# Attention levels in 64x64 quarters of the TensorE array, read from the queries themselves, and MLP operations placed ahead of the attention's in each slot

## The reference

```python
# attention: q, k, v, f_logit are (4 batches, 8 heads, 768 tokens, 48 dims)
f = sigmoid(f_logit)
for t in range(768):
    state = f[t][:, None] * state + outer(k[t], v[t])      # 48 x 48 per head
    y[t] = q[t] @ state
x = y as (3072 tokens, 384)
h = x @ w_in                                               # 384 -> 2048
g = where(h >= 1, h, where(h <= -1, 0, (h + 1)**2 / 4));  x = g @ w_out
out = (silu(x @ w_gate) * (x @ w_val)) @ w2_out            # 384 -> 1536 -> 384
```

## Time and profile before

| | |
|---|---|
| median of 3 runs | 1079.31 us (1077.73 to 1080.30) |
| the profiled execution | 1078.47 us |
| its span, first to last instruction | 1076.7 us |
| outside the span | 1.8 us |
| prologue, until the first MLP starts | 0 to 77.6 us |
| first MLP with the attention of units 1 to 5 | 77.6 to 626 us |
| second MLP | 626 to 1076.7 us |
| busy: PE, DVE, ACT, POOL | 1015.5, 547.0, 445.2, 450.8 us |

### The profile page before, as it was taken

How to read it: one execution, slowest core, us unless ns; L and a number is a source line. 1 busy time by engine, 2 the same in 40 slices (tenths; PEclk the granted TensorE clock), 3 DMA queues, 4 the chain that set the end, 5 groups by cost and what they waited for, 6 DMA issues and landing times.

```text
span 1076.7 us, 19206 instructions
## 1 busy us (share of the span) xinstructions
PE 1015.5 (94%) x7816; PEld 828.8 (77%) x7816; DVE 547.0 (51%) x745; ACT 445.2 (41%) x808; POOL 450.8 (42%) x368
## 2 busy tenths in 40 slices
PE   2477899999999999999999999999999999999997
PEld 2465677778778777877788888888888888888886
DVE  7965965884686488568736532223222222222221
ACT  3439538544753855375336532122222222222221
POOL 3956962763564476447327422121221212212121
PEclk9569999999999999999999999999999999999999
DMA  9423005003300600220043110010010010000000
GB/s 357 158 72 145 1 2 216 31 2 124 122 1 2 216 30 2 82 107 2 2 177 131 45 39 22 1 59 1 1 59 1 1 59 1 30 1 1 30 1 29
DMA packets 17367, 63.52 MB, mean 59 GB/s; under 512 B 1920, under 2 KB 2176, under 8 KB 16512
## 3 DMA queue, kind: packets, MB, share of 16 engines
q1 hardware_dynamic: 17280, 62.30, 15.8%
HBM read 52.85 MB, written 9.44 MB: 58 GB/s over the span
## 4 chain that ended last, share of the span: by engine, by line
PE 83%; issue 5%; DVE 5%; ACT 3%; POOL 3%; DMA 1%; SPq 0%; POOLq 0%; ACTq 0%; DVEq 0%
PE acc L445 10%; PE acc L447 10%; PE acc L446 10%; PE bank L473 7%; PE bank L471 7%; PE bank L472 7%; PE hid L431 6%; PE bank L344 5%; PE hid L432 5%; PE hid L433 5%; DVE scores L748 3%; PE hid L473 2%; PE hid L472 2%; PE hid L471 2%; PE bank L376 2%
## 5 line engine op out<-in xcount | busy, mean ns | idle before, releaser
L939 POOL TENSOR_TENSOR g_lo<-prod,g_hi 128x512 fp32r<-128x512 f32 x72 | 93.1, 1293 | 347.4 <-ACT g_hi L650 347.4
L932 POOL TENSOR_TENSOR g_lo<-act_tmp,g_hi 128x512 fp32r<-128x512 f32 x96 | 140.5, 1463 | 188.8 <-ACT g_hi L611 188.8
L837 DVE TENSOR_TENSOR sig<-sig,bank 128x512 f32<-128x512 f32 x72 | 49.6, 688 | 275.9 <-ACT sig L644 275.9
L748 DVE COPY_PREDICATED scores<-mask,bank 64x512 f32<-64x512 int32 x144 | 134.2, 932 | 28.4 <-PE bank L344 26.6
L650 ACT CAST g_hi<-prod 128x512 fp32r<-128x512 f32 x72 | 44.9, 624 | 247.6 <-PE acc L447 247.6
L892 POOL TENSOR_TENSOR keys<-keys,gates 128x512 f32<-128x512 f32 x82 | 110.2, 1343 | 44.1 <-PE bank L344 32.7
L611 ACT CAST g_hi<-act_tmp 128x512 fp32r<-128x512 f32 x96 | 59.6, 621 | 164.1 <-DVE act_tmp L825 164.1
L344 PEld LDWEIGHTS bank<-right_q,keys 128*64 128x64 f32 x2304 | 81.0, 150 | 58.8 <-issue 54.6
L344 PE MATMUL bank<-right_q,keys 128*64 128x64 f32 x2304 | 91.0, 238 | 36.0 <-ACT right_q L546 28.1
L445 PE MATMUL acc<-g_hi,wout_hi 128*128 128x512 f32 x288 | 117.0, 406 | 8.0 <-POOL g_lo L932 8.0
L431 PE MATMUL hid<-x_hi,win_hi 128*128 128x512 f32 x288 | 119.0, 413 | 4.0 <-DVE act_tmp L825 4.0
(11 more groups left out here) (80 smaller groups left out, 1851.6 us busy)
## 6 DMA issues: line engine op xcount, KB each, us to landing
gates<-in_f_dram SPq DMA_DIRECT2D x12, 512.0 KB, 5.3
queries<-in_q_dram SPq DMA_DIRECT2D x12, 512.0 KB, 5.4
keys<-in_k_dram SPq DMA_DIRECT2D x12, 512.0 KB, 4.7
values<-in_v_tok_dram SPq DMA_DIRECT2D x6, 1024.0 KB, 8.8
q_tok<-in_q_tok_dram SPq DMA_DIRECT2D x12, 384.0 KB, 8.6
k_tok<-in_k_tok_dram SPq DMA_DIRECT2D x12, 384.0 KB, 9.0
x_dram<-x_out SPq DMA_DIRECT2D x6, 768.0 KB, 3.9
x_raw<-x_dram SPq DMA_DIRECT2D x6, 768.0 KB, 5.5
```

Source lines behind the costliest of these rows:

```text
L748: last = dve.copy_predicated(o, level_mask(li, half), t[rows(half), :].rearrange("p (x b r) -> p x b r", x=BP, r=m))
L932: pool.tensor_tensor(g_lo[:, c % RING, :], act_tmp[:, 2 + c % 2, :], g_hi[:, c % RING, :].bitcast(F32), ALU.subtract).then_inc(g_lo_done, 1)
```

## The change

The two groups of a level become one visit: `level(a, li)` issues all 16 pairs. Each matmul now contracts over the 64 partitions of one head e, takes its weights (`keys`) and its moving columns (`queries`, every second block of m tokens, or the right half at m = 64) straight from those tensors, and writes 32 columns (64 at m = 64) of 64 partitions; head e goes to its own PSUM bank. That makes 64 matmuls a level (32 at m = 64), each in one of four 64x64 quarters of the array, in turn. `right_q`, its copies on ACT, its clearing and the semaphore `q_copied` go. `scale_q` now waits for the level's matmuls, since they read `queries`; `take_level` takes one head of all pairs rather than one group of both heads. The two last levels, whose blocks need no mask, are taken by ACT (four copies a level, 32 or 64 partitions x 512) and no longer by DVE. The levels have slots 1, 4, 7, 10, 13, 16, 18 (unit 1: 6, 9, 12, 14, 16, 18, 20), and what follows them comes one slot earlier. In each chunk `split_g1`, `activate` and `clamp` now stand before slot 2c, and `square(c)` behind slot 2c of its own chunk.

```diff
-DVE_A_UNIT, ACT_A_UNIT = STEPS + 2, B
+MASKED = 2 * (NL - 2)
+DVE_A_UNIT, ACT_A_UNIT = MASKED + 2, STEPS - MASKED + B
...
 USUAL = Plan(own=(-9, -8), diag=(-8, -7), place=(-6, -5, -4, -3), sigmoid=(-2, -1), gated=(-1, 0),
-             step=(1, 3, 5, 7, 8, 9, 10, 12, 13, 14, 15, 17, 18, 19), last_merge=21,
-             y=(21, 21, 22, 22), y_out=(21, 22, 22, 23), tk=(23, 23, 24, 24), tk_out=(24, 24, 25, 25),
-             kv=25, state=26, state_place=27)
+             level=(1, 4, 7, 10, 13, 16, 18), y=(20, 20, 21, 21), y_out=(20, 21, 21, 22),
+             tk=(22, 22, 23, 23), tk_out=(23, 23, 24, 24), kv=24, decay=21, state=25, state_place=26)
...
-        def level(a, s):
-            li, g = s // 2, s % 2
-            free(a, s)
-            pe.wait_ge(q_copied, a * STEPS + s + 1)
+        def level(a, li):
+            m = LEVELS[li]
+            for e in range(2):
+                free(a, 2 * li + e)
+            pe.wait_ge(q_scaled, a * SCALED_A_UNIT + 2 + 2 * li)
             if li:
-                pe.wait_ge(k_scaled, a * STEPS + s - 1)
+                pe.wait_ge(k_scaled, a * STEPS + 2 * li)
...
+            for x in range(BP):
+                for half in range(2 if li < NL - 1 else 1):
+                    for e in range(2):
+                        t = slice(half * HALF, (half + 1) * HALF)
+                        if li < NL - 1:
+                            o = of(a, 2 * li + e)[rows(half), x * HALF // 2:(x + 1) * HALF // 2]
+                            q_right = queries[rows(e), x, t].rearrange("p (b s r) -> p b s r", s=2, r=m)[:, :, 1, :]
...
+                        last = pe.matmul(o, keys[rows(e), x, t], q_right, start=True, stop=True)
+            last.then_inc(filled, 2)
...
-        def copy_right(a, s):
...
+        def take_level(a, li, e):      # ACT, levels m = 32 and 64
+            act.wait_ge(filled, fill(a, 2 * li + 2))
+            act.wait_ge(dve_took, a * DVE_A_UNIT + MASKED)
...
         def scale_q(a, s):
-            dve.wait_ge(q_copied, a * STEPS + s + 1)
+            dve.wait_ge(filled, fill(a, 2 * li + 2))
...
         def attention(a, h):           # DVE
-            for s in steps_at(a, h - 1):
-                take_level(a, s)
-            for s in steps_at(a, h):
-                scale_q(a, s)
+            for li in levels_at(a, h - 1):
+                if li < NL - 2:
+                    take_level(a, li, 1)
+            for li in levels_at(a, h):
+                for g in range(2):
+                    scale_q(a, 2 * li + g)
+                if li < NL - 2:
+                    take_level(a, li, 0)
...
         for m in range(UNITS):         # DVE; ACT and POOL alike
             for c in range(FC1):
-                for a, place in turns(m, 2 * c):
-                    attention(a, place)
                 if m > 0 or c > 0:
                     activate(*((m, c - 1) if c else (m - 1, FC1 - 1)))
                 clamp(m, c)
+                for a, place in turns(m, 2 * c):
+                    attention(a, place)
                 for a, place in turns(m, 2 * c + 1):
                     attention(a, place)
```

More of the change, by code:

```diff
@@ L65, with levels_at @@
 Q = P // 4
-def steps_at(a, h):
-    return [s for s in range(STEPS) if PLANS[a].step[s] == h]
+def levels_at(a, h):
+    return [li for li in range(NL) if PLANS[a].level[li] == h]
 def turns(m, h):
@@ L350, in level @@
-            last.then_inc(filled, 1)
+                for g in range(2):
+                    pe.wait_ge(k_in[g], 16 * (a + 1))
+            for x in range(BP):
[5 more added lines that the diff above has]
+                            q_right = queries[rows(e), x, t].rearrange("p (b s r) -> p b s r", s=2, r=m)[:, :, 1, :]
+                        else:
+                            o = of(a, 2 * li + e)[rows(x % 2), x // 2 * HALF:(x // 2 + 1) * HALF]
+                            q_right = queries[rows(e), x, HALF:P]
+                        last = pe.matmul(o, keys[rows(e), x, t], q_right, start=True, stop=True)
@@ L404, in attention @@
         def attention(a, h):
[L405 to L406 removed]
+            for li in levels_at(a, h):
+                level(a, li)
             for b in range(B):
@@ L526, in place_diag @@
             last.then_inc(diag_placed, 1)
-        def copy_right(a, s):
[L529 to L537, removed]
-                if li < NL - 1:
[L539 to L543, removed]
-                else:
-                    i = i[:, :, HALF:P].rearrange("p x (s t) -> p x s t", s=2)
-                last = act.copy(o, i)
-            last.then_inc(q_copied, 1)
+        def take_level(a, li, e):
+            act.wait_ge(filled, fill(a, 2 * li + 2))
+            act.wait_ge(dve_took, a * DVE_A_UNIT + MASKED)
+            t = bank[fill(a, 2 * li + e) % 3]
+            for half in range(2):
+                if li < NL - 1:
+                    r = slice(half * HALF, half * HALF + HALF // 2)
+                    o = scores[r, :, e, (2 * half + 1) * HALF // 2:(half + 1) * HALF]
+                    last = act.copy(o, t[r, :].rearrange("p (x i) -> p x i", x=BP))
+                else:
+                    o = scores[rows(0), half::2, e, HALF:P]
+                    last = act.copy(o, t[rows(half), :].rearrange("p (x i) -> p x i", x=BP // 2))
+            last.then_inc(act_took, 1)
         def take_keys(a, b):
@@ L575, in attention @@
                     sigmoid(a, g)
-            for s in steps_at(a, h + 1):
-                copy_right(a, s)
+            for li in levels_at(a, h):
+                if li >= NL - 2:
+                    for e in range(2):
+                        take_level(a, li, e)
             for b in range(B):
@@ L842, in multiply @@
             dve.tensor_tensor(prod[:, c % 2, :], s, val[c % 2][:, :], ALU.mult).then_inc(prod_done, 1)
-        for e in range(2):
-            dve.memset(right_q[rows(e), :, :, 1 - e, :].rearrange("p x s t -> p (x s) t"), 0.0).then_inc(cleared, 1)
         dve.memset(state_apart[:, :, :].rearrange("p x d -> p (x d)"), 0.0).then_inc(cleared, 1)
@@ L883, in scale_k @@
             m = LEVELS[li]
-            pool.wait_ge(filled, fill(a, s + 1))
+            pool.wait_ge(filled, fill(a, 2 * li + 2))
             if li:
@@ L905, in attention @@
                     own(a, g)
-            for s in steps_at(a, h):
-                if s < STEPS - 2 or a < UNITS - 1:
-                    scale_k(a, s)
-                if s < STEPS - 2 or 0 < a < UNITS - 1:
-                    merge(a, s)
+            for li in levels_at(a, h):
+                for g in range(2):
+                    if li < NL - 1 or a < UNITS - 1:
+                        scale_k(a, 2 * li + g)
+                for g in range(2):
+                    if li < NL - 1 or 0 < a < UNITS - 1:
+                        merge(a, 2 * li + g)
         def split_w1(i):
```

83 lines of the change are left out of this document (37 added, 46 removed).

## The result

The changed kernel takes 1089.18 us (median of 4 runs, 1088.08 to 1090.5) where the kernel before takes 1079.12 on the same chip: a ratio of 1.0094, 95% interval 1.0077 to 1.0112. It is slower by some 10 us. The spans differ by as much, 1086.3 to 1076.7, and the starts of the stages show where: the first MLP starts at 83.3 instead of 77.6 (+5.7), its first unit takes 104.4 instead of 103.7, the next four 95.4, 97.1, 97.2 and 93.0 instead of 96.0, 96.1, 96.0 and 91.3 (+3.3 in all), and from there on nothing differs.

What follows compares the result with a forecast made beforehand. PE's work bounds the units beside the first MLP, the level chain the prologue; 1078.5 - 17.0 (visits) + 19.7 (waits) + 4 (prologue) - 4.6 (order) = 1080.6, said as 1081 us; own range 1073 to 1089, 8-in-10 range 1057 to 1106.

Steps and rivals of the forecast that it cites:

- slower was the likeliest sign: Whole kernel against the one before: chances given were slower 0.45, faster 0.38, same 0.17.
- What a visit costs: PE's level visits: 2.21 us, 1.29 at m = 64; 17.0 us less for five units beside the first MLP.
- The third rival: PE's level visits: quarters don't run four at a time, 4.1 us a level, kernel about 1160; chance 0.10 with the start-rule case.
- The wait behind `scale_q`: DVE's queue: scale_q taking turns with POOL, then head 0's take, delays activate; PE waits 2.1 us at m = 1.
- The slots walked through: Slot-by-slot walk of a unit beside the first MLP: PE waits 4.05 us a unit, 16.2 for four usual units.
- The order in the slots: MLP operations ahead of the attention's: no time of their own, 4.6 us gained from late-slot waits and after 77.6.
- The prologue: Chain of levels before the first MLP: outputs worked out 5 us later at 72.3, 4 later taken.
- The 1 us taken off for a chance of the full clock: Prologue: outputs 5 us later by the working, 5 earlier if longer visits bring full clock; 4 later taken.
- The first rival: Units beside the first MLP: stalls at odd slots shrink and the visits' gain stays, 1060 us; chance 0.27.
- the mean of 0.65: Prologue of the kernel before: mean granted clock read as mostly the 1.2 GHz level, used to choose 4 us later.

Runs made afterwards that it cites:

- a3_two_places: Changed kernel with a visit's loops turned round, all of head 0 before head 1, so only two quarters take turns: 1171.55 us (one run).
- a4_q_first: Changed kernel with one added wait: POOL's scale_k of a level also waits for both scale_q of it: 1079.74 us, ratio 1.0014.
- a2_order_alone: Kernel before with only the new order, MLP operations ahead of slot 2c and square(c) in its own chunk: 1087.94 us, ratio 1.0087.
- b2_gates_early: a4_q_first with diagonal, sigmoid and gated of usual units one slot earlier, unit 1's sigmoids before three of four diagonals: 1071.43 us, ratio 0.9934.
- b4_one_diag: Changed kernel with one of eight diagonal activations left on ACT in each place of units 1 to 5: 1073.91 us (one run).
- c3_second: b2_gates_early with unit 1's last three diagonals in slots 4, 6, 7 and first two levels in slots 8 and 10: 1071.41 us, ratio 0.9931.
- b1_takes_later: a4_q_first with both takes of a level in the next slot, behind activate and clamp at odd slots: 1084.92 us, ratio 1.0062.
- c1_shift128: b1_takes_later with 128 waits more (64 instructions in the trace) at the start of PE's queue: 1084.17 us, ratio 1.0057.

## Why the prediction was right and wrong

The forecast was 1081 and the time is 1089.2, inside the range, and slower was the likeliest sign, but its own range of 1073 to 1089 was just left. Point by point:

**What a visit costs** was right: 2.21 (2.21 measured) and 1.29 (1.29). The thirty and five visits beside the MLP save 16.5 us by their medians, where 17.0 stood in the sum. The third rival, that the quarters don't run four at a time, is refuted by the 2.21; `a3_two_places` shows what two at a time cost, 3.86.

**The wait behind `scale_q`** was right in place and mechanism: 1.88 at m = 1 for the 2.1 forecast, 0.24 to 0.38 at the four other places for 0.4 to 0.6. That the two engines take turns is shown by `a4_q_first`: a wait that keeps them apart cut DVE's pair from 2.61 to 1.29 us and the wait at m = 1 by as much. The slots walked through came to 3.1 us a unit instead of 4.05, in four usual units 12.2 instead of 16.2. These 4 us too much in the sum made up for a part of what follows, which was luck.

**The order in the slots failed.** The prediction said that the MLP's operations ahead of the attention's "cost no time of their own" and booked 4.6 us of gain, half of the wait for the low part and 2 us in the startup. `a2_order_alone` puts the cost of the order at 10 us in the kernel before. In the changed kernel the wait for the low part in the late slots went from 1.3 a unit to 1.24 and not to 0.65, `gated` now stood behind `activate` and `clamp` and made the first visit 1.24 late, and unit 1's first level comes 7.0 us late (5.2 of them idle, the rest its own visit at the 1.2 GHz level). The queue of ACT was named as crowded, but its way to PE through `gated` was not followed: the visit now needs the second group's queries too, and those come last. (In `a2_order_alone` the first visit is 1.26 late although it needs the first group alone, so this is not the whole of it.) What the five units beside the first MLP lost again is 3.9 (the difference in stage time) + 16.5 = 20.4 us, where 19.7 - 4.6 = 15.1 was forecast. Some 4 of them are no idle time but PE at the 1.2 GHz level behind two waits of unit 1; the sum had no term for that.

**The prologue** was right and its size set too low: 5.7 instead of 4. Its visits all took what they take at the 1.2 GHz level:

```profile
28.18 3.64 PE L353 MATMUL bank<-queries,keys 64*64 64x32 f32 x128 [5.26 <-DVE scores L744]
37.25 3.62 PE L353 MATMUL bank<-queries,keys 64*64 64x32 f32 x128 [5.43 <-DVE scores L744]
44.84 3.64 PE L353 MATMUL bank<-queries,keys 64*64 64x32 f32 x128 [3.98 <-DVE scores L744]
```

The levels follow each other by 8.9, 9.1, 7.6, 7.5, 7.5 and 6.9 us (9.2, 7.7 and 7.1 forecast), PE waiting for the take that frees the bank (for `scale_k` before the last), and the outputs start at 72.65, by the working 72.3. That is two misses which cancel: the last level started at 66.71, 1 us earlier than worked out, and the outputs came 5.9 us behind it instead of 4.6. The 1 us taken off for a chance of the full clock should have stayed.

So 16.5 saved, 20.4 lost beside the MLP and 5.7 in the prologue: +9.6, the difference of the spans. The first rival's gain is seen in `b2_gates_early`: the visits' saving is real and stays once those waits are out of the way. Unit 1's first wait goes with most of ACT's diagonals (`b4_one_diag`) and with the sigmoids ahead of them (`b2_gates_early`); what is left in that unit, waits for the low part or for POOL's `scale_k`, was only moved about (`c3_second`).

## What to carry to other kernels

Before a faster step replaces a decoupling copy, list what stands in the queue of the engine that now waits, and who wants it: here a saving of 3.3 us a unit was real and was paid back by waits of 0.3 to 1.9 us, most of which an added wait and one slot's change in the plan removed. Where two engines take turns, let the one on the critical path go first, even by an added wait. An order that one version needs may cost another version as much as it gives this one, so measure a reordering alone. And count the granted clock with the waits: behind a long one PE's next microseconds can cost double.

## What was not expected of the hardware

**A dense visit can outrun its instructions.** A visit is 256 instructions (128 loads, 128 matmuls) in 2 us. In `b1_takes_later`, `c1_shift128` and five other variants PE stopped for 0.8 to 2.0 us, always at number 193 of a run of 256 of its queue or the one beside it, and the profile puts it down to "issue". The trace's DMA records show instruction fetches of 16 KB, 82 of them for the 20972 instructions of PE's queue (62 for 15995 in the kernel before), so one for 256. They tie the stops to the fetches: each of the 18 stops in the seven variants ends 1.2 to 1.4 us after the end of a fetch. Matched in order, one fetch to one run, number 193 of a run starts in no trace less than 1.2 us behind the end of its fetch, in the kernel before and the changed kernel neither. The changed kernel itself has no such stop beside its MLP; where waits were removed stops appeared, and they ate the gain of `b1_takes_later`. What decides when a block is fetched was not found.

**The granted clock of the prologue can't be taken from a window.** The changed kernel shows 0.73 from 19.3 to 72.9, `a4_q_first` the following:

```profile
20.00:75.00 55.00, 26.10 (x868) 25.31 (x867) 32.03 (x37) 9.16 (x14) 40.19 (x36) 1.00 0.33 128
```

It is 1.00, the 2.4 GHz level, and yet its visits there last 3.64 us as in the changed kernel, against 2.07 later. The clock's records in the trace begin only at 76.1 us in `a4_q_first` and at 40.7 in the changed kernel, and the view counts what lies before the first record as full. The 0.73 hides the same:

```profile
19.30:40.70 21.40, 10.71 (x384) 10.47 (x384) 15.58 (x12) 3.33 (x4) 14.53 (x10) 1.00 0.87 338
44.10:72.90 28.80, 13.14 (x456) 12.69 (x460) 18.98 (x21) 6.20 (x10) 27.34 (x24) 0.50 0.01 2
```

The visits of 128 records last 3.62 to 3.64 us in both stretches. So the mean of 0.65 that the prediction read in the earlier trace rows is a mean over such a gap too (the kernel before has its first record at 24.4), and in the prologue the duration of the visits is the better witness.
